# Windowed attention in front of two expert layers: weighted products of two units in a row, and sums of squares in one tile of high and low parts

## The reference

```
rms = sqrt(mean(x * x, axis=-1) + 1e-6);  xn = x / rms * rms_g
y   = (silu(xn @ w_gate) * (xn @ w_val)) @ w_out        # 512 -> 1536 -> 512
```

## Time and profile before

| | |
|---|---|
| median of three runs | 810.62 us |
| the profiled execution: its time, its span | 810.14 us, 808.2 us |
| PE busy | 799.2 us, 99% |
| weight loads busy | 719.6 us, 89% |
| DVE, ACT, POOL busy | 60%, 38%, 25% |
| from 60 to 80 us: PE, DVE, ACT busy | 19.97, 18.24, 18.02 of 20 us |
| DMA engines busy from 20 to 60 us | 93 to 94% |
| chain that ended last | PE 96% |

### The profile page before, as it was taken

The page is one execution under the profiler, slowest core; times in us unless marked ns, Lnnn a source line. Parts: engine busy times, 40 slices in busy tenths (PEclk is TensorE's granted clock), DMA queues, the critical chain, the costliest instruction groups (busy, mean ns, idle before and its releaser), DMA issues.

```text
span 808.2 us, 14997 instructions
## 1 busy us (share of the span) xinstructions
PE 799.2 (99%) x4797; PEld 719.6 (89%) x4798; DVE 488.0 (60%) x993; ACT 305.8 (38%) x667; POOL 205.3 (25%) x187
## 2 busy tenths in 40 slices
PE   9999999999999999999999999999999999999996
PEld 8999999999999999999999999988888888888885
DVE  7989645667657764857586667736226445564352
ACT  7989743121321132121213123435324534543341
POOL 5565995040004000500130000051920110110100
PEclk9999999999999999999999999999999999999999
DMA  7998950020002002000200013326353643755100
GB/s 223 303 316 285 339 228 1 1 78 1 1 1 79 0 1 75 6 1 1 79 0 1 1 40 105 111 77 217 136 187 131 249 155 130 258 188 199 55 15 26
DMA packets 42720, 86.88 MB, mean 107 GB/s; under 512 B 6494, under 2 KB 16990, under 8 KB 42144
## 3 DMA queue, kind: packets, MB, share of 16 engines
q1 hardware_dynamic: 36144, 75.41, 26.8%
q0 software_dynamic: 3360, 10.40, 3.8%
q10 hardware_dynamic: 3152, 0.26, 0.3%
HBM read 72.54 MB, written 14.30 MB: 107 GB/s over the span
## 4 chain that ended last, share of the span: by engine, by line
PE 96%; DMA 1%; issue 1%; DVE 1%; ACT 1%; SPq 0%; ACTq 0%; POOLq 0%; DVEq 0%
PE ps L1126 28%; PE ps L1128 28%; PE ps L1127 28%; PE ps L1059 3%; PE ps L1275 2%; PE ps L1094 2%; PE ps L1079 1%; PE ps L1193 1%; DMA kt<-kT 1%; PE ps L1053 1%; ACT pr L795 0%; PE ps L1035 0%; DMA out<-osb,sidx 0%; PE ps L1303 0%; DVE nmax L1430 0%
## 5 line engine op out<-in xcount | busy, mean ns | idle before, releaser
L1126 PE MATMUL ps<-xn_hi,GV_hi 128*128 128x384 f32 x576 | 194.2, 337 | 0.0
L1128 PE MATMUL ps<-xn_hi,GV_lo 128*128 128x384 f32 x576 | 193.4, 336 | 0.0
L1127 PE MATMUL ps<-xn_lo,GV_hi 128*128 128x384 f32 x576 | 192.9, 335 | 0.0
L1126 PEld LDWEIGHTS ps<-xn_hi,GV_hi 128*128 128x128 f32 x576 | 108.2, 188 | 2.8
L1127 PEld LDWEIGHTS ps<-xn_lo,GV_hi 128*128 128x128 f32 x576 | 108.2, 188 | 2.7
L1128 PEld LDWEIGHTS ps<-xn_hi,GV_lo 128*128 128x128 f32 x576 | 108.1, 188 | 0.0
L853 ACT ACTIVATE h_hi<-ps 128x384 fp32r<-128x384 f32 x72 | 35.5, 493 | 160.8 <-DVE ps L1520 159.0
L1550 DVE CUSTOM_DVE_ANT_0 ps<-ysb,wrb 128x512 f32<-128x512 f32 x120 | 92.2, 769 | 6.0 <-ACT ysb L860 1.0
L847 ACT ACTIVATE sig<-ps 128x384 f32<-128x384 f32 x71 | 35.0, 493 | 159.9 <-PE ps L1128 140.7
L1128 PE MATMUL ps<-Wo_hi,h_lo 128*128 128x512 f32 x216 | 85.5, 396 | 0.0
L1127 PE MATMUL ps<-Wo_lo,h_hi 128*128 128x512 f32 x216 | 85.3, 395 | 0.0
(11 more groups left out here) (185 smaller groups left out, 1363.3 us busy)
## 6 DMA issues: line engine op xcount, KB each, us to landing
EW_raw<-w SPq DMA_DIRECT2D x32, 1024.0 KB, 7.6
vt<-vW SPq DMA_DIRECT2D x16, 512.0 KB, 5.2
y_rows<-ysb SPq DMA_DIRECT2D x6, 768.0 KB, 3.9
kt<-kT SPq DMA_DIRECT2D x47, 96.0 KB, 4.6
qraw<-qT SPq DMA_DIRECT2D x15, 288.0 KB, 4.1
xraw<-xT_rows SPq DMA_DIRECT2D x5, 768.0 KB, 5.4
xT_rows<-xo SPq DMA_DIRECT2D x12, 288.0 KB, 3.5
raw_out<-w_out SPq DMA_DIRECT2D x3, 1024.0 KB, 7.9
```

The source lines that it names most:

```text
L1126: nc.tensor.matmul(out, a_hi, b_hi, start=start, stop=False)
L1127: nc.tensor.matmul(out, a_hi, b_lo, start=False, stop=False)
L1128: return nc.tensor.matmul(out, a_lo, b_hi, start=False, stop=stop)
```

## The change

- `pt` becomes two tiles, one for each parity; the copies into it wait for the products of the unit before the last instead of the last (`o_ready` at n - 1).
- In pairs 1 to 6 PE leaves out `weighted` in the even unit and makes the products of both units, 2p-2 and 2p-1, one after the other in the odd unit, behind block 0. They write to three banks, 5 to 7. In pair 7 (`closing`) and after it the order of single products stays.
- In pairs 1 to 6 ACT copies both results in the odd unit: behind the exponentials of block 1 and of block 2.
- Bank 7 no longer has room for DVE's reciprocals of block 1; they go to spare columns of the block's own score bank, so that scores of block 1 now wait for the normalisation of job j-3, not for its exponentials.
- SP's order in attention is written anew for pairs: the first keys before the stores, the values of the even unit behind the first keys of the odd unit, and those of the odd unit behind its other keys.
- Sums of squares: GpSimd adds the upper 64 lanes of `ssq` onto the lower, and writes the rounded value to the lower half of one tile and the remainder to the upper (`fold_squares`, four operations on 64 lanes in place of two on 128). PE multiplies one tile once, for the first chunk too. Its fold stands in unit 11, and its product moves from before the transposition of block 0 of unit 15 to behind that of block 1.

```diff
 def squared(c):
-    return (2 * KD - 1) * (c + 1) + 2 * c
+    return (2 * KD - 1 + FOLDS) * (c + 1)
...
@@ SP @@
+            for pair in range(1, UNITS // 2 - 1):
+                n = 2 * pair
+                if pair > 1:
+                    queries_keys(n, 0, True, lambda: store_of(n - 4)(n - 4, 0))
+                    store_of(n - 3)(n - 3, 1)
+                else:
+                    queries_keys(n, 0)
+                if pair <= KEPT:
+                    load_half(pair - 1, 0)
+                else:
+                    load_quarter(pair - KEPT - 1, 0)
+                queries_keys(n + 1, 1, pair < UNITS // 2 - 2, lambda: load_v(n, 0))
+                load_v(n + 1, 1)
...
@@ GpSimd @@
+            def fold_squares(base):
+                low, high = slice(0, P // 2), slice(P // 2, P)
+                at = base + 2 * KD - 1
+                g.tensor_tensor(sq[low], ssq[high], ones_r[high, 0:1].bitcast(F32).to_broadcast([P // 2, CH]), ALU.mult).then_inc(sq_step, 1)
+                pool.wait_ge(sq_step, done(at + 1))
+                g.tensor_tensor(ssq[low], ssq[low], sq[low], ALU.add).then_inc(sq_step, 1)
+                pool.wait_ge(sq_step, done(at + 2))
+                g.tensor_tensor(ssq_parts[low], ssq[low], ones_r[low, 0:1].bitcast(F32).to_broadcast([P // 2, CH]),
+                                ALU.mult).then_inc(sq_step, 1)
+                pool.wait_ge(sq_step, done(at + 3))
+                g.tensor_tensor(ssq_parts[high], ssq[low], ssq_parts[low].bitcast(F32), ALU.subtract).then_inc(sq_step, 1)
+                pool.wait_ge(sq_step, done(at + FOLDS))
...
@@ ACT @@
             def move_pt(n, u):
-                act.wait_ge(o_ready, done(n))
+                act.wait_ge(o_ready, done(n - 1))
...
                     exps(j, u, b)
-                    if b == 0:
-                        copy_o(2 * pair + u - O_LAG, u, 16 * pair, kept)
+                    if closing and (u, b) in ((0, 1), (1, 0)):
+                        copy_o(2 * pair - O_LAG + u, u, 16 * pair)
+                    elif not closing and u == 1 and b > 0:
+                        n = 2 * pair - O_LAG + b - 1
+                        copy_o(n, b - 1, 16 * pair, isinstance(pair, int) and n < PAIRS, 2 - b)
...
@@ PE, mean_squares and first_mean_squares @@
-                nc.tensor.matmul(ps[:, MISC, 0:CH], ones_r[:], ssq_hi[:], start=True, stop=False)
-                nc.tensor.matmul(ps[:, MISC, 0:CH], ones_r[:], ssq_lo[:], start=False, stop=True).then_inc(misc_ready, 1)
+                nc.tensor.matmul(ps[:, MISC, 0:CH], ones_r[:], ssq_parts[:], start=True, stop=True).then_inc(misc_ready, 1)
...
-                nc.tensor.matmul(ps[:, SUMS_BANK, 0:CH], ones_r[:].bitcast(F32), ssq[:], start=True, stop=True).then_inc(misc_ready, 1)
+                nc.tensor.matmul(ps[:, SUMS_BANK, 0:CH], ones_r[:], ssq_parts[:], start=True, stop=True).then_inc(misc_ready, 1)
...
@@ PE, scores @@
-                pe.wait_ge(exp_ready, done(j - 2))
+                pe.wait_ge(p_ready if b == 1 else exp_ready, done(j - 2))
...
@@ PE, pair_of_units @@
                     scores(j, n, u, b, 16 * pair + 16)
                     weights_T(n - 1, 1 - u, b)
-                    if b == 0:
+                    if b == 0 and closing:
                         weighted(n - O_LAG, u, 16 * pair)
+                    elif b == 0 and u == 1:
+                        weighted(2 * pair - O_LAG, 0, 16 * pair)
+                        weighted(2 * pair - O_LAG + 1, 1, 16 * pair, True)
...
@@ PE, attention_end @@
-                first_mean_squares()
                 weights_T(UNITS - 1, 1, 0)
                 half_gate(c, 0, par, *gv_weights[0], range(1, 2))
                 weighted(UNITS - 2, 0, 8 * UNITS)
                 weights_T(UNITS - 1, 1, 1)
+                first_mean_squares()
...
@@ DVE, normalize @@
                 if b == 1:
-                    bank = MISC
+                    bank = S_BANK + b
...
@@ DVE, copy_pt @@
-                dve.wait_ge(o_ready, done(n))
+                dve.wait_ge(o_ready, done(n - 1))
```

More of the change, by code:

```diff
@@ L78 @@
 LEAD = 6
+FOLDS = 4
 def done(k):
@@ L219, in build @@
         pr = [r.take(f"pr{u}", NBLK, KEYS) for u in range(2)]
-        pt = r.take("pt", JOBS, BPJ * P)
+        pt = [r.take(f"pt{u}", JOBS, BPJ * P) for u in range(2)]
         den = [r.take(f"den{u}", NBLK) for u in range(2)]
@@ L230, in build @@
         rms = ssq
[L231 to L232 removed]
+        ssq_parts = Region(squares_at).take("ssq_parts", CH, dt=F32R)
         wrb_at = squares_at - 4 * E * D
@@ L453, in _, with queries_keys, store_of @@
             load_keys(3, 1)
-            def unit(n, u, q=True, k=True, half=None, quarter=None, store=store_xT):
-                store(n - 2, u)
+            def queries_keys(n, u, q=True, between=None):
                 if q:
                     load_q(n + 3, 1 - u)
[L459 to L478, removed]
+                load_k(n + 2, u, 0)
+                if between is not None:
+                    between()
+                load_keys(n + 2, u, range(1, JOBS))
+            def store_of(n):
+                return store_rest if n < PAIRS else store_xT
+            for pair in range(1, UNITS // 2 - 1):
[11 more added lines that the diff above has]
+                load_v(n + 1, 1)
+                if pair <= KEPT:
+                    load_half(pair - 1, 1)
+                else:
+                    load_quarter(pair - KEPT - 1, 1)
+            store_xT(UNITS - 6, 0)
+            load_v(UNITS - 2, 0)
+            store_xT(UNITS - 5, 1)
+            load_v(UNITS - 1, 1)
+            store_xT(UNITS - 4, 0)
+            store_xT(UNITS - 3, 1)
             load_wo(0)
@@ L660, in _ @@
             square_at = {9: (0, 1), 10: (2, 3)}
-            scale_at = {14: range(KD)}
+            fold_at, scale_at = 11, {14: range(KD)}
             for n in range(3, UNITS):
@@ L669, in _ @@
                     square(0, xc0, square_at[n])
+                if n == fold_at:
+                    pool.wait_ge(qbd_ready, done(2 * n + 2))
+                    fold_squares(0)
                 for k in scale_at.get(n, ()):
@@ L820, in _, with pair_of_units @@
                 exps(j, u, b)
-            def pair_of_units(pair, kept=False):
+            def pair_of_units(pair, closing=False):
                 for j, u, b in jobs(2 * JOBS * pair, 2 * JOBS):
@@ L832, in _ @@
             for pair in range(1, KEPT + 1):
-                pair_of_units(pair, True)
-            with act.Fori(KEPT + 1, UNITS // 2) as pair:
                 pair_of_units(pair)
+            with act.Fori(KEPT + 1, UNITS // 2 - 1) as pair:
+                pair_of_units(pair)
+            pair_of_units(UNITS // 2 - 1, True)
             def root(c, bank=MISC):
@@ L1081, in weights_T, with weighted @@
                 last.then_inc(pt_ready, 1)
-            def weighted(n, u, loads):
+            def weighted(n, u, loads, paired=False):
                 pe.wait_ge(pt_copied, done(2 * n + 2))
@@ L1110, in _, with pair_of_units @@
                     weights_T(u - 1, u - 1, b)
-            def pair_of_units(pair):
+            def pair_of_units(pair, closing=False):
                 for j, u, b in jobs(2 * JOBS * pair, 2 * JOBS):
@@ L1115, in pair_of_units @@
                     weights_T(n - 1, 1 - u, b)
-                    if b == 0:
+                    if b == 0 and closing:
                         weighted(n - O_LAG, u, 16 * pair)
-            with pe.Fori(1, UNITS // 2) as pair:
+                    elif b == 0 and u == 1:
+                        weighted(2 * pair - O_LAG, 0, 16 * pair)
+                        weighted(2 * pair - O_LAG + 1, 1, 16 * pair, True)
+            with pe.Fori(1, UNITS // 2 - 1) as pair:
                 pair_of_units(pair)
+            pair_of_units(UNITS // 2 - 1, True)
             def three(out, a, b, start, stop):
```

20 lines of the change are left out of this document (9 added, 11 removed).

## The result

The changed kernel takes 814.56 us (median of 6 runs, 813.79 to 816.78), the kernel before beside it 811.13 (6 runs, 810.16 to 811.32): a ratio of 1.0044, interval 1.0033 to 1.0054, slower by 3.4 us. The profiled executions took 813.97 us with a span of 812.2 and 810.14 us with a span of 808.2.

The account below looks back on a forecast made before the run. PE and the chain through the single pt were taken as even before, ACT's chain as binding after. Terms +0.4, +2.8, +0.6, -0.55, -0.6 and -0.85, together +1.8, gave 812.4 us from 810.62; range 808.2 to 815.

Parts of the forecast that it names:

- First pair, +0.4: First pair of attention units: scores of block 1 wait for the normalisation three jobs back; +0.4 us, between -0.24 and +0.6.
- Five pairs at 10.1, +2.8: The five pairs after the first take 10.1 us each instead of 9.54, adding 2.8 us.
- less covered stalls, -0.55: PE's new idle time covers part of the 1.14 us of old stalls in attention: -0.55, bounds 0 and -1.14.
- ACT's chain: Loop once per pair through PE, DVE and ACT's exponentials and both copies: sum 10.03 us, taken as 10.1.
- The new wait beside the chain: Scores of block 1 waiting for the normalisation three jobs back cost time only in the first pair.
- Closing pair, +0.6: Last pair keeps the old order but finds ACT late: two units of 5.07 us, 10.14 together, +0.6.
- First sum -0.6: First sum of squares on PE: one pass of 0.17 us replaces an fp32 product of 0.75; gain 0.58, rounded.
- Five later sums, 0.85: Five later sums of squares on PE each lose one of two passes, 0.17 us each: 0.85 us saved.
- GpSimd's fold at no cost: GpSimd's four operations on 64 lanes add 0.2 to 2.3 us, covered by at least 5 us: cost 0.
- The rival that had the products wait for late values: Odd unit's values, issued behind two key loads, land late: 815 us if 1 us late in half the pairs; chance 0.15.
- PE's own 9.30: PE's work alone per pair, 9.30 us; rival that PE binds and not ACT's chain: 807.7 us, chance 0.15.
- the old 9.54: Pair length before the change; rival that pairs stay there and only sums of squares count: 809.2 us, chance 0.10.

Follow-up runs that it names:

- experiment 4: Changed kernel with block 1's reciprocals in SBUF, so its scores wait for exponentials only: 815.36 us, 1.0058 of the kernel before.
- experiment 2: Changed kernel with one more copy of 576 columns out of PSUM on ACT, ahead of a pair's first copy: 818.65 us, 1.0094 of the kernel before.
- experiments 3, 4 and 6: Changed kernel with ACT's copies moved (816.34, 814.96, 816.77 us); block 1's reciprocals in SBUF (815.36); copies moved and stores first (815.33, 815.37, 815.45).

## Why the prediction was right, and where it was not

The range of 808.2 to 815 and the sign, slower, hold 814.56, but by 0.4 us only. The forecast's own range, 810.9 to 814, doesn't, and of the change the sum had about half: +1.8 for 3.4 in the medians and 4.0 in the spans. By its steps, which add up to the 4.0:

- **First pair, +0.4**: +1.05 in this execution. It has two waits for DVE at the new semaphore (0.64 and 0.53), the kind foreseen, and one for keys at 16.94 (1.03), which wasn't. In the six kernels of the experiments with the same scores and waits where the keys hold that mask back by 0.24 or less, the first double product starts at 17.32 to 17.86, here at 18.20: without the keys +0.2 to +0.7. So the 0.47 of experiment 4 can't be called the wait's price.
- **Five pairs at 10.1, +2.8, less covered stalls, -0.55**: the starts span 50.56 for 47.70, +2.86. Stalls were 1.03 before and are 0.32 now (the last double product, whose values landed late): -0.71. The two sets take 2.25 as summed, so PE's own gain is there; it is covered. The number is right, the mechanism half, and that 10.1 met 10.11 is in part luck: the chain that decides isn't the one that was summed. The terms of ACT's chain came out as summed: 1.04, 0.53, 0.37, 1.02 and 0.53 in ACT's lines, and 1.69 idle ahead of (B,1) for "some 1.5". But the prediction went through DVE by its waits for data, as if it were free each time, and not through its queue. The earlier trace rows held each duration for that chain of 9.98, which stays when the copies go. By experiment 2 alone ACT would have been called the cause. The rule of the Trainium skill on copying out of PSUM (TensorEngine Tiling (Array Packing), "PSUM Bottleneck") pointed at ACT as well; the runs give its copies 0.13 a pair.
- **The new wait beside the chain**: right in the pairs, by 0.21 us (9.77 to 9.98).
- **Closing pair, +0.6**: +2.23. This is the term that was mis-sized, by 1.6 of the 2.2 that the sum lacks. Its second unit took 5.16 (78.05 to 83.21) for a forecast 5.07. The first took 6.72, because the product of unit 12 shares a bank with the result of unit 11 and waits for its copy, which starts at 76.01, behind the exponentials (B,2). But values for it weren't there either: in five kernels with a copy moved it waits 1.63 to 1.90 for them, and starts 0.2 to 0.3 behind their landing. In the kernel after they were issued at 72.74 and landed at some 76.3, for a start at 76.85. So SP's order would have cost nearly as much in the same place, all but 0.2 to 0.3 (an estimate from these landings): one wait hides the other.
- **First sum -0.6**: -0.86 with its change of place. The pass itself holds PE 0.26 (88.56 to 88.82) for 0.75; in the kernel with the sums alone the same stretch, from the mask at 78.49 to the products at 87.96, is 0.56 shorter than before. The other 0.3 came with the attention part and isn't explained. **Five later sums, 0.85**: four gave 0.61 to the start of the fifth, 0.15 each. **GpSimd's fold at no cost**: right, PE never waited for it.

The rival that had the products wait for late values is in part true: in the kernel after they cost 0.32 at the last double product and would hold the closing pair, and with shorter pairs they came too late in several (up to 6.6 to land, where the prediction left 5.5 for 5.2). PE's own 9.30 and the old 9.54 were not reached in any pair of the ten kernels with double products.

What stays open: kernels with double products seem to scatter more (6 runs over 3.0 us for the kernel after and 5.1 with both copies early and stores first, 1.2 for the 6 of the kernel before; over the 13 to 17 runs beside the experiments it is 2.4 to 3.2). Two things could do it, and the traces hold one execution each: values that land late in some, and the clock. In five of the seven kernels of experiments 3, 4 and 6 the slowest run has the lowest mean granted clock of its kernel, 0.996 where most have 0.998 or 0.999. Nor was it tried to take work off DVE.

## What to carry to other kernels

When two engines' work is regrouped, walk round the loop once for each engine that works in order, adding its whole queue between two of its waits, not only the operations on the data's path: here three such loops lay within 0.13 us a pair. A dose added to one loop (a copy more) shows that it is close to binding, not that relief will pay; only taking it away shows what is next. And look at the last turn of a regrouped loop by itself: of the 5.43 us that attention lost, 1.87 were one wait where the old order takes over, with a second reason for nearly the same wait behind it.

## What the runs showed of the hardware

- **Half the lanes of GpSimd save nothing.** The fold's lines, ns as min, median and max:

```profile
L637 POOL TENSOR_TENSOR ssq_parts<-ssq,ones_r x6: 818/820/821, 56.7 to 414.7; 64x384 fp32r<-64x384 f32 x6
L640 POOL TENSOR_TENSOR ssq_parts<-ssq,ssq_parts x6: 996/1341/1345, 57.6 to 415.6; 64x384 fp32r<-64x384 f32 x6
```

The subtraction on 128 lanes took 1.02, on 64 it takes 1.00 in the first fold and 1.34 at the median; the multiplication on 128 lanes took at least 0.83, on 64 it takes 0.82. The Trainium skill (GPSIMD Engine Reference, "Instruction dispatch") has each of eight cores work on its own 16 partitions, by which idle lanes would save no time; the rows agree.

- **A multiplication on DVE with all operands in SBUF** took 0.56 us or up to 1.01, with the reciprocals in PSUM always 0.55. Of the sixteen, nine took 0.68 to 1.01, each with a GpSimd arithmetic operation under way at its start. Of the seven of 0.56, three (8.98, 17.71, 27.99) had no GpSimd operation beside them, one (13.35) short ones that only write (IOTA); at 59.05 and 87.21 GpSimd began one 0.02 later, and at 69.33 one was under way. The Trainium skill (GPSIMD Engine Reference, "Key points") says that the two engines share SBUF interfaces and that DVE instructions with two SBUF inputs contend with GpSimd. The nine long ones agree with it; the last three of 0.56 show that it doesn't strike each time.
- **TensorE's clock fell behind the two longest waits.** Behind idle times of 2.41 and 2.02 before the product of unit 12 it was granted 0.50 for some 3 us; behind waits of 1.63 to 1.90 in the same place, in the other eight kernels with double products, it stayed at 1.00. The price, by the product of unit 12 to that of unit 13: 6.38 and 6.34, against 5.02 to 5.98 in the others.
- **Copies out of PSUM in a row on ACT** start 0.53 apart (576 columns) and 0.37 (384), though each is 0.66 and 0.51 long.
